# Sums of the ending's output weights split five and three over two phases, low parts of the first Silu form a unit sooner, and one bank's sum ahead of three low parts

## The reference, cut to what matters

```python
# attention with keys and values pooled by 8; q, k, v: (4, 8, 576, 64)
attn = softmax(q @ pool8(k).T / 8) @ pool8(v)
x = attn.transpose(0, 2, 1, 3).reshape(2304, 512)
# first FFN
xn = x / sqrt(mean(x * x) + 1e-6) * rms_g
g = xn @ w_gate                       # 512 x 1536
x = (g * sigmoid(g) * (xn @ w_val)) @ w_out
# second FFN
h = x @ w_in                          # 512 x 2048
out = (h * sigmoid(h)) @ w2_out       # 2048 x 512
```

## Time and profile before

| what | value |
|---|---|
| median of three runs | 876.26 us |
| the profiled execution | 876.44 us |
| its span | 874.7 us |
| TensorE (PE) busy | 858.8 us, 98% |
| DVE, ACT, POOL busy | 64%, 41%, 49% |
| granted clock of TensorE | 1.000 |
| DMA | 235.78 MB, 269 GB/s over the span |

### The profile page before, as it was taken

The page is one execution under the profiler, slowest core; times in us unless marked ns, Lnnn a source line. Parts: engine busy times, 40 slices in busy tenths (PEclk is TensorE's granted clock), DMA queues, the critical chain, the costliest instruction groups (busy, mean ns, idle before and its releaser), DMA issues.

```text
span 874.7 us, 13955 instructions
## 1 busy us (share of the span) xinstructions
PE 858.8 (98%) x5328; PEld 837.7 (96%) x5328; DVE 561.8 (64%) x846; ACT 355.1 (41%) x643; POOL 430.5 (49%) x433
## 2 busy tenths in 40 slices
PE   7999999999999999999999999999999999999898
PEld 6999999999999999999899899999999999999898
DVE  6689757766556766656554355679633898334973
ACT  3689745542222233346553122126233534234431
POOL 6898999882347571657773054330352700001600
PEclk9999999999999999999999999999999999999999
DMA  9971678778899994656779389986598948688562
GB/s 251 253 229 39 228 274 320 279 297 313 310 326 353 361 349 150 242 198 258 272 298 369 144 311 372 366 315 265 211 336 325 338 158 282 262 305 274 201 243 104
DMA packets 85249, 235.78 MB, mean 270 GB/s; under 512 B 22848, under 2 KB 53568, under 8 KB 73024
## 3 DMA queue, kind: packets, MB, share of 16 engines
q1 hardware_dynamic: 85184, 234.90, 74.8%
HBM read 159.39 MB, written 75.50 MB: 269 GB/s over the span
## 4 chain that ended last, share of the span: by engine, by line
PE 83%; DMA 6%; POOL 5%; DVE 3%; issue 2%; SPq 1%; ACT 0%; POOLq 0%; DVEq 0%; ACTq 0%
PE ps L1987 15%; PE ps L1989 15%; PE ps L1988 15%; DMA fold_home<-fb 4%; PE ps L2120 4%; PE ps L2122 4%; PE ps L2121 4%; PE ps L1914 3%; PE ps L2026 3%; PE ps L2028 3%; PE ps L2027 3%; PE ps L2053 3%; PE ps L2052 3%; PE ps L2051 2%; DVE efl L1653 2%
## 5 line engine op out<-in xcount | busy, mean ns | idle before, releaser
L1987 PE MATMUL ps<-xh,wr 128*128 128x384 f32 x840 | 282.6, 336 | 0.1
L1989 PE MATMUL ps<-xh,wr 128*128 128x384 f32 x840 | 281.3, 335 | 0.0
L1988 PE MATMUL ps<-xl,wr 128*128 128x384 f32 x840 | 281.1, 335 | 0.0
L1987 PEld LDWEIGHTS ps<-xh,wr 128*128 128x128 f32 x840 | 157.7, 188 | 3.1 <-DVE qt L1561 0.9
L1988 PEld LDWEIGHTS ps<-xl,wr 128*128 128x128 f32 x840 | 157.8, 188 | 0.3
L1989 PEld LDWEIGHTS ps<-xh,wr 128*128 128x128 f32 x840 | 157.7, 188 | 0.0
L2120 PE MATMUL ps<-ew,efh 128*128 128x256 f32 x336 | 95.8, 285 | 5.7 <-DVE xacc L1679 3.0
L2121 PE MATMUL ps<-ew,efh 128*128 128x256 f32 x336 | 95.1, 283 | 0.0
L2122 PE MATMUL ps<-ew,efl 128*128 128x256 f32 x336 | 95.1, 283 | 0.0
L957 POOL TENSOR_TENSOR eh<-eh 128x768 f32<-128x768 f32 x8 | 18.6, 2350 | 117.0 <-DVE efl L1653 117.0
L1580 DVE TENSOR_TENSOR qt<-ps,qt 128x384 f32<-128x384 f32 x84 | 46.0, 555 | 42.1 <-PE ps L1989 41.9
(11 more groups left out here) (198 smaller groups left out, 1738.9 us busy)
## 6 DMA issues: line engine op xcount, KB each, us to landing
wr<-ring_home SPq DMA_DIRECT2D x40, 1792.0 KB, 9.2
ring_home<-wr SPq DMA_DIRECT2D x20, 1792.0 KB, 8.1
ew<-ending_home SPq DMA_DIRECT2D x8, 2048.0 KB, 8.1
out_home<-wo SPq DMA_DIRECT2D x14, 1024.0 KB, 9.4
ew<-out_home SPq DMA_DIRECT2D x24, 512.0 KB, 6.8
fw<-fold_home SPq DMA_DIRECT2D x7, 1536.0 KB, 6.4
ending_home<-eb SPq DMA_DIRECT2D x16, 512.0 KB, 10.6
raw_c<-in_moe_w_out SPq DMA_DIRECT2D x13, 512.0 KB, 7.8
```

Source lines behind the costliest of these rows:

```text
L1987: pe.matmul(out_ps, w_hi, x_hi, start=first and c == 0, stop=False, skip_group_check=True)
L1988: pe.matmul(out_ps, w_hi, x_lo, start=False, stop=False, skip_group_check=True)
L1989: ins = pe.matmul(out_ps, w_lo, x_hi, start=False, stop=c == 1, skip_group_check=True)
```

## The change

It does four things. The eight sums of the ending's weights are placed anew: five (`CEARLY`) are made on POOL before phase 3's hidden differences and three after `whole`, with another order of the two buffers (`CHOME`: three sums in buffer 1, five in buffer 0), and SP keeps them at other units. `load_ending(0, 0)` waits for buffer 1's stores alone and stands one unit sooner; the wait for buffer 0's moves to the next two loads. The high and low parts of product 0's form stand at the ends of the units 5 and 6 of an ending phase (counted from 0), where they stood at 6 and 7. In `dve_ending` the sum c11 of tile 0 comes after one low part of product 2 where it came after two.

```diff
--- before.py
+++ after.py
@@ -220,8 +220,9 @@
 
     MADE = len(made)
     made += [("c", j) for j in range(2 * EPART)]
-    CHOME = [1, 0, 1, 0, 0, 1, 0, 1]
-    C_AT = {first_unit[(WHOLE, WHOLE + 1)[j // EPART]] + (2, 4, 6, 7, 0, 2, 3, 4)[j]: j for j in range(2 * EPART)}
+    CHOME = [1, 0, 1, 0, 0, 0, 1, 0]
+    CEARLY = 5
+    C_AT = {first_unit[WHOLE + (j >= CEARLY)] + (2, 4, 6, 7, 9, 0, 1, 3)[j]: j for j in range(2 * EPART)}
     c_before = [max((m for m in range(j) if CHOME[m] == CHOME[j]), default=None) for j in range(2 * EPART)]
     c_store = [32 * sum(1 for m in range(j + 1) if CHOME[m] == CHOME[j]) for j in range(2 * EPART)]
     made_at = {m: i for i, m in enumerate(made)}
@@ -573,7 +574,7 @@
                     sp.wait_ge(s_vsum, 3)
                 if made[i] == ("r", U2 + 1):
                     sp.wait_ge(s_bst, 16 * 2 * PART)
-                if made[i] == ("c", 5):
+                if made[i] == ("c", 6):
                     sp.wait_ge(s_wh, 2 * NF)
                 if kind in "ab":
 
@@ -596,7 +597,7 @@
             def keep(i):
 
                 kind, x = made[i]
-                if raw_next[i] is not None and made[raw_next[i]] not in (("r", U2 + 1), ("c", 5)) \
+                if raw_next[i] is not None and made[raw_next[i]] not in (("r", U2 + 1), ("c", 6)) \
                         and made[raw_next[i]][0] != "b":
                     load_raw(raw_next[i])
                 sp.wait_ge(s_wlo, i + 1)
@@ -645,11 +646,11 @@
                 f, done = EPRODUCTS[i][1], ET * NF * e
                 if i == 0 and e == 0:
                     sp.wait_ge(s_wh, 2 * NF)
-                    sp.wait_ge(s_cst[1], 32 * EPART)
-                    sp.wait_ge(s_cst[0], 32 * EPART)
+                    sp.wait_ge(s_cst[1], 32 * CHOME.count(1))
                 elif i == 0:
                     sp.wait_ge(s_end, done)
                 elif i < 3:
+                    sp.wait_ge(s_cst[0], 32 * CHOME.count(0))
                     sp.wait_ge(s_prod, NF * (last_unit[ENDINGS[e]] + i - 1))
                 elif i == 5:
 
@@ -749,11 +750,11 @@
                 if item == ("unit", first_unit[WHOLE] + 1):
                     load_raw(made_at["c", 1])
                 if item == ("whole", WHOLE):
-                    load_raw(made_at["c", 5])
+                    load_raw(made_at["c", 6])
                 if kind == "unit" and x in C_AT:
                     keep(made_at["c", C_AT[x]])
                 for e, ph in enumerate(ENDINGS):
-                    if item == ("unit", last_unit[ph] - 2):
+                    if item == ("unit", last_unit[ph] - 3):
                         load_ending(e, 0)
                     if item == ("unit", last_unit[ph] - 1):
                         load_ending(e, 1)
@@ -1056,7 +1057,7 @@
                 else:
                     fold_sums(i)
 
-            for j in range(EPART):
+            for j in range(CEARLY):
                 ending_weight_sums(made_at["c", j])
             first_group = downs.index((WHOLE, 0))
             for j in range(PART):
@@ -1064,7 +1065,7 @@
             for j in range(PART):
                 hidden_sums(5, j)
             pool.wait_ge(s_wh, 2 * NF)
-            for j in range(EPART, 2 * EPART):
+            for j in range(CEARLY, 2 * EPART):
                 ending_weight_sums(made_at["c", j])
             for e in range(2):
                 for f in (3, 5):
@@ -1360,9 +1361,8 @@
                         silu(x, i)
                 if ph == WHOLE and (letter, g) == ("G", PART):
                     form_high(0)
-                if ph in ENDINGS and g >= 2 * EPART - 2:
-                    i = g - 2 * EPART + 2
-                    ending_high(ENDINGS.index(ph), 0, range(2 * i, 2 * i + 2))
+                if ph in ENDINGS and g - EPART in (1, 2):
+                    ending_high(ENDINGS.index(ph), 0, ((0, 1), (2, 3))[g - EPART - 1])
                 if ph in ENDINGS and x == last_unit[ph]:
                     ending_high(ENDINGS.index(ph), 1, range(EPART - 1))
 
@@ -1647,7 +1647,7 @@
                 for j in parts:
                     dve.wait_ge(s_ehi, EPART * (NF * e + i) + j + 1)
                     if i == 0 and e == 0:
-                        dve.wait_ge(s_cst[0], 32 * EPART)
+                        dve.wait_ge(s_cst[0], 32 * CHOME.count(0))
                     elif i == 1:
                         dve.wait_ge(s_prod, NF * (last_unit[ENDINGS[e]] + 1))
                     dve.tensor_tensor(efl[e][i % 2][:, 2 * j:2 * j + 2, :], ending_part(f, j),
@@ -1680,9 +1680,9 @@
 
             def dve_ending(e):
                 ending_low(e, 1)
-                ending_low(e, 2, (0, 1))
+                ending_low(e, 2, (0,))
                 ending_sum(e, "c11", 0)
-                ending_low(e, 2, (2, 3))
+                ending_low(e, 2, (1, 2, 3))
                 for j in range(EPART):
                     ending_hidden_sums(e, 4, j)
                 ending_sum(e, "c11", 1)
@@ -1774,9 +1774,8 @@
                         low(n, 0)
                 if ph == WHOLE and 2 * PART + 1 <= x - first_unit[ph] <= 3 * PART:
                     form_low(0, [x - first_unit[ph] - 2 * PART - 1])
-                if ph in ENDINGS and g >= 2 * EPART - 2:
-                    i = g - 2 * EPART + 2
-                    ending_low(ENDINGS.index(ph), 0, range(2 * i, 2 * i + 2))
+                if ph in ENDINGS and g - EPART in (1, 2):
+                    ending_low(ENDINGS.index(ph), 0, ((0, 1), (2, 3))[g - EPART - 1])
 
             dve.memset(KV[0][0][LAST:P, RC - 1, :], 0.0).then_inc(s_pad0, 1)
             for i in range(2):
```

## The result

The changed kernel takes 867.94 us (median of five runs, 867.12 to 869.04), against 875.87 us (875.19 to 876.70) for the kernel before on the same chip: a ratio of 0.991, 95% interval 0.990 to 0.993, or 6.4 to 8.9 us less. The profiled execution took 869.04 us, where 869.3 was forecast for it.

What follows compares the result with a forecast made beforehand. TensorE, busy 98% of the span, was taken to bound the kernel. 876.44 less 7.3 for the endings' breaks plus 0.2 gave 869.3 profiled; less 0.18, the forecast was 869.2 us, range 868.4 to 872.0.

Steps and rivals of the forecast that it cites:

- The six breaks: TensorE's idle gaps in both endings: 1.48, 0.26, 1.67, 0.25, 1.34, 1.67 us, plus 0.6 for restarts; 7.3 to win.
- Part 1: Endings: product 0's low parts a unit sooner, leaving POOL three differences instead of six at 685.7; cost 0.0 to 0.1 each.
- Part 2: Endings: sum c11 ahead of three low parts, done 697.1 to 698.9, bank wanted at 699.5; credited with 1.67 us twice.
- the 1.67 goes, twice: In each ending, TensorE's 1.67 us wait for the DVE sum c11 before product 1's third tile was to vanish.
- Part 3: First ending: weight load `ew` issued at 663.7, 13 us sooner, waiting only for the other buffer's stores; 1.48 us wait goes.
- Part 4: Weight sums on POOL placed five and three, in the whole phase and before the endings; cost taken as 0.
- (a): Before the first ending: the last sum's store lands at 668.6, DVE asks for it at 671.2; margin 2.6 us.
- (b): Whole phase: POOL's fifth sum ends at 573.5, six differences by 586.4; cost 0, cover 3 us.
- (c): Folded product: store and raw load precede product 1's fold load, landing 587.5, wanted 589.3; loss 0 to 2.0, taken 0.
- The first rival: Product 1's fold load comes late, costing up to 2.0 us: 869.3 to 871.3; chance 0.12.
- the lock inside the unit: Ending phases' units: a POOL difference slows DVE's low-part pair, 2.52 us each, 6.4 in both endings: 875.6; chance 0.04.
- the slower case: Whole phase starves behind late fold loads: break even at a 596.6 landing, 0.2% slower (878.0) from 598.4; chance 0.04.

Runs made afterwards that it cites:

- the changed kernel's second time: The changed kernel measured again with no edit: median 867.60 us, ratio to the kernel before 0.989 to 0.992.
- its third: The changed kernel measured once more with no edit: median 868.29 us, ratio to the kernel before 0.991 to 0.994.
- one edit: Kernel before with only the high and low parts of product 0 a unit sooner: 869.78 us, ratio 0.992 to 0.995.
- another: Kernel before with only the sum c11 of tile 0 ahead of one more low part: 872.72 us, ratio 0.995 to 0.998.
- a third: Changed kernel with the sooner low parts and the sum c11's move undone, leaving weight sums and load: 874.82 us, ratio to before 0.998 to 1.000.
- The pair of 3.62 us inside the unit: Changed kernel with POOL's first difference of each ending waiting for unit 6's second Silu: 871.47 us, ratio to before 0.994 to 0.996.
- no copy, one or three: Changed kernel with extra copies of the fifth sum's store (1 MB each) ahead of product 1's fold load: one 869.76 us, three 878.28; none 867.94.

## Why the prediction was right or wrong

**The sum.** Forecast was 7.3 less 0.2; the three traces show 7.4. The six breaks are gone, the restarts with them, and the 0.1 put on each ending for the low parts inside the units is 0.0: the pair at 671.14 is through when the combination at 672.88 can begin. In the profiled execution, 869.3 forecast stands against 869.04.

**The step that failed** is the last one, "the median before lies 0.18 below the profiled one, so 869.2", and with it the lower end of the range, "no residue at the unit ends, a matmul restart saved". Together they leave the spread of executions those 0.18 us, taken from one comparison of three runs, and anchor the rest on one trace. The stretch ahead of the folded product takes 580.6 to 583.2 us, and the 582.87 of the trace of before lies near the slow side of that. Medians of the same kernel before were 875.87, 875.93, 875.51 and 875.23 in the four comparisons, 0.3 to 1.0 us below the 876.26 that the forecast started from, and medians of the same changed kernel 867.6 to 868.3. The 1.2 us between 869.16 (869.2 as it was rounded) and 867.94 are made up of 0.4 from that start (876.26 against 875.87), 0.3 from the sum (7.4 against 7.1) and 0.5 of spread between the two kernels' medians (7.9 against 7.4). A range for this kernel needed 1 us below the forecast for executions alone, whatever the change does.

**Part 1** stands in time: POOL was through with its first two differences at 676.5 (675.6 forecast; it starts when DVE's first piece is done, at 672.1, not at 671.3), had about three left at 685.7, and DVE's four pieces ended at 694.1 (694.2 forecast). One reading was wrong: the "2.15 for the two at 679.40" is no time of POOL alone but a mean. The first of the two took 2.50 us beside a low part, the second 1.85 alone. That changed nothing in the sum.

**Part 2** came out in time, but its credit was wrong. The forecast wrote "the 1.67 goes, twice" under it. Without it the 1.67 goes just the same. The working of that part had the numbers to say so: product 1's pieces end at 694.2, two pieces of product 2 would end at 696.9, the bank is wanted at 699.5.

**Part 3**: the load went out at 663.81 (663.7 forecast) and the 1.48 went. That it could be won at all was owed to part 1, which the sum of six breaks hid; alone it gained 0.0. The credit to the narrower wait was also misplaced: the sooner last store does it. The size, 1.48, is one draw from losses of 0.8 to 1.9 us (start to start).

**Part 4**: (a) DVE did not wait at 671.14. (b) POOL's fifth sum ended at 574.4 (573.5 forecast), its differences by 583.5 and the last, after the final gate, from 585.05. (c) The fold load landed at 586.6 (587.5 forecast) and nothing was lost. The term at 0 was right, but with less cover than this one trace shows. There the load was in time by 2.6 us (wanted at 582.92 + 6.25 = 589.2). In the six other traces with the same sums and no copies it landed 0.5 to 1.5 us before its need: at 587.8 against 588.5 in the changed kernel's second time, at 588.0 against 589.5 in its third. The first rival was that near.

**The rivals.** The fold load that comes late, the lock inside the unit and the slower case all exist as mechanisms and were made to happen by edits; in the changed kernel none of them occurs. The late load cost 1.1 us for a landing 1.1 us past its need, one for one as worked out. The lock cost 3.6 us and not 6.4: only the second piece of a pair waits for a whole difference (1.11 and 2.58 us, not twice 2.52). The slower case had a price too low: with a landing at 595.5 the kernel was already slower than before (ratio 1.002 to 1.004), where the forecast had it break even at 596.6, since the load was wanted 2.4 us sooner and a break of 8.7 us also brought a lower clock.

## What to carry to other kernels

When an engine is busy all the time but for a few breaks, work out each break's next limit before adding them up: here one edit was worth 5.4 us alone, another 3.0 alone and 0.0 beside the first, a third 0.0 alone and 1.1 or more beside it. Two engines that take turns on the same memory are best parted in time, and the operations to move are those that let the other engine start sooner. And give the range the spread of executions first: two traces of unchanged code, cut at the same instruction, show it.

## What the runs showed of the hardware

- A DVE operation with two operands in SBUF and a POOL difference take turns, and both pay. Alone, the difference takes 1.84 us and DVE's low part 0.95; side by side they take 2.56 and 2.60. It is so in the changed kernel too, where the merged rows above give only the means of four (2.17 and 2.10). Its single rows, from the timelines of POOL and DVE:

```profile
685.51 1.84 POOL L962 TENSOR_TENSOR eh<-eh 128x768 f32<-128x768 f32 x1
687.33 2.56 POOL L962 TENSOR_TENSOR eh<-eh 128x768 f32<-128x768 f32 x1
```
```profile
690.62 2.60 DVE L1653 TENSOR_TENSOR efl<-eh,efh 128x768 fp32r<-128x768 f32 x1
693.15 0.95 DVE L1653 TENSOR_TENSOR efl<-eh,efh 128x768 fp32r<-128x768 f32 x1
```

- The Trainium skill (SBUF — State Buffer, the section on the two separate sides of SBUF) says that whichever starts first has the port pair for the whole instruction and the other is fully blocked. The pair of 3.62 us inside the unit agrees. Its first low part starts 0.3 us before a difference ends and takes 1.11; the second starts while the next difference runs, which ends at 680.0, and takes 2.58, about 1.8 of it in front of that end; and that difference, begun beside the first low part, takes 2.57 instead of 1.84:

```profile
677.46 2.57 POOL L960 TENSOR_TENSOR eh<-eh 128x768 f32<-128x768 f32 x1
```
```profile
677.22 1.11 DVE L1655 TENSOR_TENSOR efl<-eh,efh 128x768 fp32r<-128x768 f32 x1
678.26 2.58 DVE L1655 TENSOR_TENSOR efl<-eh,efh 128x768 fp32r<-128x768 f32 x1
```

- SP's queue itself is held up under load. Two 512 KB stores were issued in 1.01 us; the two copies after them took 2.68 us, and six took 9.12. The fold load behind them landed 10.6 to 11.1 us after its issue in every kernel with the fifth sum's store ahead of it, with no copy, one or three (7.8 in the kernel before, without that store), so the delay of the copies showed in the time of issue, not in the landing.
- In the break of 8.56 us TensorE's granted clock fell: it was 1.00 up to 590, with no matmul since 587, and 0.50 from 591 on. Behind the break TensorE ran for about 5 us with starts 0.32 us apart, close to half its rate, at the lower of its two levels (1.2 GHz); from 601 the clock was 1.00 again. Behind breaks of up to 1.7 us it stayed at 1.00.
